# The first expert of an attention-and-experts kernel: six staging buffers for w1, token gathers right behind them, DVE makes the low halves

## The reference

```python
def _attn_ref(r, k, v, w, u):                 # B, H, S, D = 4, 8, 768, 48
    for t in range(S):
        kt, vt, rt = (k[:, :, t], v[:, :, t], r[:, :, t])
        cur = np.einsum('bhd,bhe->bhde', u[None] * kt, vt)
        y[:, :, t] = np.einsum('bhd,bhde->bhe', rt, state + cur)
        state = w[None, :, :, None] * state + np.einsum('bhd,bhe->bhde', kt, vt)

def _moe_ref(x, w_gate, w1, w2):              # N, D, E, F = 3072, 384, 8, 1024
    cap = N // E
    flat = (x @ w_gate).flatten()
    for idx in np.argsort(-flat):
        tok, e = (int(idx) // E, int(idx) % E)
        if assigned[tok] >= 0 or counts[e] >= cap:
            continue
        assigned[tok] = e
        counts[e] += 1
    for e in range(E):
        mask = assigned == e
        out[mask] = np.maximum(x[mask] @ w1[e], 0.0) @ w2[e]

def _moe2_ref(x, w_a, w_b, w_out):            # d_ff = 1536
    return (x @ w_a) * (x @ w_b) @ w_out
```

## Time and profile before

| | us |
|---|---|
| median of 3 executions | 904.5 |
| lowest and highest | 902.1, 906.38 |
| profiled execution, its own time | 903.44 |
| its span, first to last instruction | 901.5 |
| PE busy, share of the span | 831.6, 92% |
| DVE, ACT, POOL busy | 538.3, 234.6, 425.8 |

### The profile page before, as it was taken

One profiled execution on the slowest core, in us unless ns is written; L12 is line 12 of the kernel. 1 busy time (PEld: TensorE's weight loads), 2 busy tenths in 40 slices (PEclk: granted clock), 3 DMA queues, 4 the chain that ended last, 5 costly groups with the idle time before them and its releaser, 6 DMA issues.

```text
span 901.5 us, 19288 instructions
## 1 busy us (share of the span) xinstructions
PE 831.6 (92%) x7941; PEld 798.6 (89%) x7941; DVE 538.3 (60%) x1294; ACT 234.6 (26%) x494; POOL 425.8 (47%) x448
## 2 busy tenths in 40 slices
PE   5898987329999999999999999999999999999994
PEld 5798887219999999999999999999999999999994
DVE  6675765657776676677657675777576422631221
ACT  2233322021223123312322232223222222331221
POOL 5666764067047605751673177217622770475001
PEclk9999999559999999999999999999999999999998
DMA  9997951031012102210121122012101220121000
GB/s 171 204 226 169 223 134 47 1 113 55 1 59 80 55 1 71 77 46 14 66 79 37 36 65 67 27 36 80 54 27 36 88 59 12 60 82 53 1 1 27
DMA packets 94023, 61.82 MB, mean 69 GB/s; under 512 B 79344, under 2 KB 83952, under 8 KB 93936
## 3 DMA queue, kind: packets, MB, share of 16 engines
q0 software_dynamic: 11008, 34.61, 12.5%
q1 hardware_dynamic: 78640, 21.25, 11.9%
q10 hardware_dynamic: 4288, 4.72, 1.5%
HBM read 51.13 MB, written 9.44 MB: 67 GB/s over the span
## 4 chain that ended last, share of the span: by engine, by line
PE 76%; DVE 3%; issue 1%; DMA 1%; POOL 1%; ACT 0%; ACTq 0%; POOLq 0%; DVEq 0%
PE bank L1252 41%; PE bank L1326 17%; PE bank L1295 11%; PE bank L1308 2%; PE bank L1275 2%; PE bank L1312 1%; DVE mask_mem L682 1%; PE bank L1192 1%; DMA wst<-in_moe_w,rows_i 1%; PE bank L1243 1%; PE bank L1208 1%; PE bank L1200 1%; PE bank L1233 0%; POOL w L502 0%; DVE cand L678 0%
## 5 line engine op out<-in xcount | busy, mean ns | idle before, releaser
L1252 PE MATMUL bank<-act,w_all 128*128 128x384 f32 x1584 | 295.9, 338 | 0.0
L1252 PEld LDWEIGHTS bank<-act,w_all 128*128 128x128 f32 x1584 | 275.3, 188 | 0.0
L485 POOL DMA_INDIRECT wst<-in_moe_w,rows_i x48 | 52.3, 1090 | 246.3 <-DVE rows_i L752 190.9
L1326 PE MATMUL bank<-w_all,gs 128*128 128x384 f32 x864 | 167.4, 337 | 0.3 <-DVE gs L875 0.3
L502 POOL TENSOR_TENSOR w<-wst,w 128x384 fp32r<-128x384 f32 (+1 forms) x106 | 130.6, 1232 | 43.9 <-ACT w L1016 38.2
L1326 PEld LDWEIGHTS bank<-w_all,gs 128*128 128x128 f32 x864 | 150.0, 188 | 0.6 <-DVE gs L875 0.6
L1295 PE MATMUL bank<-hs,w 128*128 128x384 f32 x576 | 113.1, 340 | 0.0
L872 DVE TENSOR_TENSOR ga<-ga,bank 128x384 f32<-128x384 f32 x96 | 53.0, 552 | 86.2 <-PE bank L1252 80.6
L1295 PEld LDWEIGHTS bank<-hs,w 128*128 128x128 f32 x576 | 100.6, 188 | 0.0
L1037 ACT ACTIVATE gs<-ga 128x384 fp32r<-128x384 f32 x96 | 50.5, 526 | 187.2 <-DVE ga L872 187.2
L1252 PE MATMUL bank<-act,w 128*128 128x384 f32 x504 | 98.5, 339 | 0.0
(11 more groups left out here) (179 smaller groups left out, 1047.0 us busy)
## 6 DMA issues: line engine op xcount, KB each, us to landing
kt<-in_k SPq DMA_DIRECT2D x24, 192.0 KB, 4.1
rt<-in_r SPq DMA_DIRECT2D x24, 192.0 KB, 4.7
vt<-in_v SPq DMA_DIRECT2D x24, 192.0 KB, 4.9
x_rows<-xs ACTq DMA_DIRECT2D x24, 192.0 KB, 3.4
raw<-in_moe_w_a SPq DMA_DIRECT2D x6, 384.0 KB, 4.8
raw<-in_moe_w_b SPq DMA_DIRECT2D x6, 384.0 KB, 5.3
raw<-in_moe_w_out SPq DMA_DIRECT2D x6, 384.0 KB, 5.2
wst<-in_moe_w,rows_i POOLq DMA_INDIRECT x112
```

The source lines that it names most:

```text
L485: pool.indirect_dma_start(wst[:, k % STAGES, :], None, w1_rows, bass.IndirectOffsetOnAxis(ap=rows_i[:, k:k + 1], axis=0)).then_inc(wst_lan ...
L1252: last = pe.matmul(dst, wt(a), mv(b), start=(n == 0 and (a, b) == (0, 0)), stop=(n == len(pairs) - 1 and (a, b) == (1, 0)))
L1326: last = pe.matmul(acc[t][:, 0:D], gs2[:, c % 2, a, t * P:t * P + P], wo2[:, b, c, :], start=(c == 0 and (a, b) == (0, 0)), stop=(c == FFC ...
```

## The change

- `parts_of` gives blocks k = 3, 4, 5 of expert 0 staging buffers of their own: two stretches of `os_` and one of `ga`, with their own semaphores (`spare_landed`). Expert 0 thus has six buffers for its w1 blocks. The blocks of w2 go to `wst` as before; k = 6, 7, 8 wait for the low halves of 0, 1, 2.
- POOL's work for expert 0 is a function of its own, `prepare_first`: 16 increments of the semaphore `pool_go` (`PAD`), the wait for the row numbers, six gathers of w1, the three token gathers, then the gathers of w2, with POOL's halves of k = 8 on.
- DVE makes the low halves of k = 0 to 7 (before: 2 to 7): 0 to 5, then `route_keys(1)` and `lower_tokens(0)`, then 6 and 7. ACT's upper halves of the tokens come after k = 5 (before: after 4).
- The last three instructions of `route_places` become `route_close`, called ahead of `route_ids`, for every expert.
- DVE's two memsets after the attention stand ahead of the wait for the logits. In the last step of the attention ACT copies the logits of tile 22 ahead of the store of tile 23.

The diff, with what is only renamed left out:

```diff
+        spare_landed = [sem(f"spare_landed{n}") for n in range(STAGES)]
...
-        TOKENS_AT_0, TOKENS_AT = 4, 6
+        TOKENS_AT = 6
...
-        BY_DVE, BEFORE_TOKENS = range(2, 8), range(2, 5)
+        BY_DVE, BEFORE_TOKENS = range(0, 8), range(0, 6)
...
+        os_flat = os_[:, :, :].rearrange("p t d -> p (t d)")
+        spare = [os_flat[:, 0:WIDE], os_flat[:, WIDE:2 * WIDE],
+                 ga[:, :, :].rearrange("p q t -> p (q t)")[:, 0:WIDE]]
+        def in_spare(m, k):
+            return m == 0 and STAGES <= k < W1C
...
             def gather_weights(m, k):
-                if k >= STAGES:
+                if m == 0 and W1C <= k < W1C + STAGES:
+                    pool.wait_ge(w_split, 1 + (k - W1C + 1))
+                elif k >= STAGES and not in_spare(m, k):
                     pool.wait_ge(w_split, 1 + (m * CHUNKS + (k - STAGES + 1)))
                 else:
                     pool.wait_ge(w_split, 1 + m * CHUNKS)
...
+            def prepare_first():
+                for _ in range(PAD):
+                    pool.sem_inc(pool_go, 1)
+                pool.wait_ge(rows_ready, 1)
+                for k in range(W1C):
+                    gather_weights(0, k)
+                gather_tokens(0)
+                for k in range(W1C, CHUNKS + 2):
+                    if k < CHUNKS:
+                        gather_weights(0, k)
+                    if k - 2 > BY_DVE[-1]:
+                        split_weights(0, k - 2)
...
             dve.wait_ge(s_cpool, CP_ALL + 1)
-            dve.wait_ge(lg_ready, NT)
             dve.memset(is_open[:, :], 1.0)
             dve.memset(lid[:, :], BIG).then_inc(hole_step, 1)
             dve.wait_ge(hole_step, 1)
+            dve.wait_ge(lg_ready, NT)
...
+            def route_close(m):
                 dve.tensor_tensor(is_open[:, :], is_open[:, :], member[:, :], ALU.subtract)
                 link(m, dve.tensor_scalar(chosen[:, :], chosen[:, :], -2.0 * BIG, None, ALU.mult))
...
                     if more and c == 4 + PARTS:
+                        route_close(i + 1)
                         route_ids(i + 1)
...
             for part in range(PARTS):
                 route_slots(0, part)
+            route_close(0)
             route_ids(0)
             for k in BY_DVE:
                 if k == BEFORE_TOKENS[-1] + 1:
                     route_keys(1)
                     lower_tokens(0)
-                if k == BY_DVE[0]:
-                    dve.wait_ge(w_split, 1 + k)
...
                 upper_raw(n)
+                if n == NT - 1:
+                    copy_logits(n - 1)
                 store(n)
                 if n + 1 < NT:
                     copy_sums(n + 1)
-                if n >= 1:
+                if 1 <= n < NT - 1:
                     copy_logits(n - 1)
...
+PAD = 16
```

More of the change, by code:

```diff
@@ L325, in parts_of, with landings, landed @@
                 c, o = k * WIDE // F, k * WIDE % F
-                return wst[:, s, :], w1_2[:, 0, c, o:o + WIDE], w1_2[:, 1, c, o:o + WIDE]
+                return (spare[s] if in_spare(m, k) else wst[:, s, :],
+                        w1_2[:, 0, c, o:o + WIDE], w1_2[:, 1, c, o:o + WIDE])
             return wst[:, s, 0:D], w2_2[:, 0, k - W1C, :], w2_2[:, 1, k - W1C, :]
+        def landings(m, k):
+            s = k % STAGES
+            if m == 0:
+                return 16 * (k // STAGES if k >= W1C else 1)
+            return 16 * (m * len(range(s, CHUNKS, STAGES)) - 1 + k // STAGES + 1)
+        def landed(m, k):
+            return spare_landed[k % STAGES] if in_spare(m, k) else wst_landed[k % STAGES]
         CP_IDENT, CP_CAUSAL, CP_ALL = 4, 9, 29
@@ L502, in split_weights, with gather_tokens, prepare @@
                 pool.tensor_tensor(lo, src, hi.bitcast(F32), ALU.subtract).then_inc(w_split, 1)
-            def prepare(m, first):
+            def gather_tokens(m):
+                pool.wait_ge(ids_ready, m + 1)
+                pool.wait_ge(xg_turned, 1 + m * DC)
+                pool.sem_inc(pool_go, 1)
+                for t in range(CT):
+                    pool.indirect_dma_start(xg[:, t, :], None, x_rows,
+                                            bass.IndirectOffsetOnAxis(ap=ids_next[:, t:t + 1], axis=0)
+                                            ).then_inc(xg_landed[t], 16)
+            def prepare_first():
+                for _ in range(PAD):
+                    pool.sem_inc(pool_go, 1)
+                pool.wait_ge(rows_ready, 1)
[7 more added lines that the diff above has]
+                        split_weights(0, k - 2)
+            def prepare(m):
                 pool.wait_ge(rows_ready, m + 1)
@@ L510, in prepare @@
                         gather_weights(m, k)
[L511 to L518, removed]
-                                                    bass.IndirectOffsetOnAxis(ap=ids_next[:, t:t + 1], axis=0)
-                                                    ).then_inc(xg_landed[t], 16)
+                    if k >= 2:
+                        split_weights(m, k - 2)
+                    if k == TOKENS_AT:
+                        gather_tokens(m)
             def store(i):
@@ L530, in store @@
                 pool.sem_inc(o_flushed, 1)
[L532 removed]
+            prepare_first()
             for i in range(E - 1):
[L534 removed]
+                prepare(i + 1)
                 store(i)
@@ L1010, in upper_weights @@
             def upper_weights(m, k):
-                s = k % STAGES
-                uses = len(range(s, CHUNKS, STAGES))
-                act.wait_ge(wst_landed[s], m * (16 * uses) + 16 * (k // STAGES + 1))
-                src, hi, lo = parts_of(k)
+                act.wait_ge(landed(m, k), landings(m, k))
+                src, hi, lo = parts_of(m, k)
                 act.activation(hi, src, ACT.Copy).then_inc(w_hi, 1)
```

27 lines of the change are left out of this document (13 added, 14 removed).

## The result

| | before | after |
|---|---|---|
| median, us | 904.56 (4 executions) | 899.21 (4 executions) |
| lowest and highest | 902.1, 906.38 | 898.99, 900.08 |
| profiled execution, its span | 903.44, 901.5 | 899.0, 897.0 |

The ratio is 0.9944, 95% interval 0.992 to 0.9969: 5.35 us, 0.6%, faster. The forecast was 898.9 in a range of 896.8 to 901.6.

The account below looks back on a forecast made before the run. TensorE's back-to-back expert work bounds the kernel, so gains lie ahead of the first product: 0.65 + 0.13 + 0.54 + 4.28 = 5.60 us off the 904.5 median gives 898.9, range 896.8 to 901.6.

Parts of the forecast that it names:

- What bounds: TensorE busy 677.82 of 680 us in the experts; time saved ahead of the first product comes off the end nearly whole.
- Rival D: Expert 0: the start moves but the gain is lost to late w2 halves or search lists; 904 us, chance 0.05.
- Parts 1 and 2: End of attention: last logit copy ahead of the last store saves 0.65 us, memsets ahead of the logit wait 0.13.
- Part 3: First routing: `route_close` moved behind the third one-hot takes 0.54 us off the path to the token numbers.
- Part 4: POOL, before expert 0's first gather: 16 increments move a code load into idle time; row numbers to gather 1.08, not 3.69.
- Rival A: POOL's pad does nothing and the stall stays: tokens 1.22 us later, gain 4.4, 900.1 us; chance 0.20.
- Part 5: Expert 0's gathers: six buffers and new order bring the third token gather 5.60 us earlier, 4.28 from POOL's queue.
- Does DVE disturb the gathers?: POOL's six w1 gathers: even stretched by 0.19 or 0.23 us each beside DVE instructions, no cost.
- Third token gather to first product: Landing, transposes and halves of the tokens before expert 0's first product: taken as fixed at 4.93 us.
- B: Rival: w1 landings bunch, binding from 1.75 us spacing; at 1.89 costs 0.7 us, 899.6 us; chance 0.09.
- C: Rival: w1 blocks and tokens share DMA engines, landing over 2.9 us apart; slower, 907 us at 3.4; chance 0.04.
- The clock: First product: TensorE's clock rises 3.2 us after dense work; at once wins 1.6 us, twice as long loses 1.6.

Follow-up runs that it names:

- pad0: Changed kernel without the 16 semaphore increments on POOL (PAD = 0): median 899.20 us, ratio to before 0.9985.
- pad1: Changed kernel with one semaphore increment on POOL instead of 16: 896.55 us, one execution.
- pad129: Changed kernel with 129 semaphore increments on POOL instead of 16: 895.98 us, one execution.
- psum_numbers: Changed kernel with the first routing's one-hots reading the slot numbers from a PSUM bank instead of SBUF: median 896.52 us, ratio to before 0.9945.
- close_back: Changed kernel with route_close(0) back ahead of the one-hots of the first routing: 894.65 us, one execution.
- after: The changed kernel itself, against the kernel before: median 899.21 us, ratio 0.9944.
- after_again: The changed kernel, unedited, measured and profiled again: median 897.21 us, ratio to before 0.993.
- pad128: Changed kernel with 128 semaphore increments on POOL instead of 16: 900.42 us, one execution.
- warm: Changed kernel with token gathers ahead of gather k=5, plus some 120 extra identity matmuls on TensorE in the first routing: median 903.07 us, ratio to before 0.9995.

## Why the prediction was right, step by step

- **What bounds.** Held: 678.62 of 680 us busy, and the time ahead of the first product came off the end. Rival D (lost in expert 0) is out.
- **Parts 1 and 2**, 0.78: 0.80 measured, where the clock is high at the end of the attention. The profiled execution of the changed kernel has nothing of it.
- **Part 3**, 0.54: from row numbers to the end of `ids_next` it is 9.32 instead of 10.00, so 0.68, of which 0.31 is the last instruction itself (0.16 instead of 0.47), which I hadn't forecast. The one-hots do start 0.54 sooner. What counts is less, at most some 0.2, because the token gathers didn't wait for these numbers alone.
- **Part 4**, the pad: 1.23 from row numbers to first gather against 1.08 predicted, and the cause was right. **Its price was the worst term.** Rival A gave 1.22 for a pad without effect; it is 3.9. The step that failed is "POOL is free at 186.7, a microsecond before the token numbers": its sixth gather ended at 188.77, and these were ready at 187.34.
- **Part 5**, 4.82 with part 3: the measured 4.27 falls short by 0.55, and the token gathers are where. I had the first 0.85 behind `ids_next`; it was 1.73, since two gathers were held (0.83 and 1.02 above 0.95) and the sixth ended 1.43 us after the token numbers. From the first token gather to the third it was 2.51, not 2.69, and the numbers themselves came 0.14 sooner: 0.88 - 0.18 - 0.14 = 0.56. "Does DVE disturb the gathers?" was answered from gathers that stood beside short instructions; the one-hots of 1.2 us, to which the change moved the gathers, were not among them.
- **Third token gather to first product**, taken as fixed at 4.93: 4.92.
- **The landings** (B and C): they didn't bunch. The sixth block was in ACT's hands 3.56 us after its gather's start (187.57 to 191.13), the first 3.67, and from the first to the sixth it is 8.21 us at ACT and 8.32 at the issue, with unequal steps between. That is 1.64 a block, not the 1.28 I had counted on and not far from the 1.75 at which B binds, but it comes from the held gathers. So k=5 came at 191.13 and not 189.4, the keys ended at 194.70 and not 193.2, and the spare time before the tokens' lower half was 1.1 and not 2.2.
- **The clock**: it rose some 5.3 us after the first product's start, not 3.2. The 2.1 us more at half speed are worth about 1.05, within the 1.6 I gave; the end shows 0.74 more. The other traces say that the clock has less to do with it: where it rose 3.0 to 3.5 us after the first product's start (`pad0`, `pad1`, `pad129`, `psum_numbers`, `close_back`) it is 700.1 to 700.5 from there to the end, where it rose 5.3 to 5.5 after (`after`, `after_again`, `pad128`) 700.5 to 700.7. What makes the rest of the 0.74 stays open.
- **The number**: luck had a part. Both errors go the same way, 0.55 less gained before the first product and 0.74 lost behind it, and the profiled pair shows 4.50 and not 5.60. That the medians differ by 5.35 is the scatter of whole executions, so the time was met closer than the terms deserve.

## What to carry to other kernels

Two changes that both shorten one queue are priced together: in the trace the one alone took 2.11 us off the way to the first product, the other 0.39, both 4.27, since the second only pays once the first has emptied the queue ahead of it. (In whole times each alone was 0.15%, no more than noise, and both 0.6%.) When work is moved, look at which long two-input VectorE instructions it will then stand beside, not at what it stood beside before. A stall in "issue" just ahead of a gather may be a load of that engine's code. The signs here were a packet of the engine's instruction queue inside the stall, and a stall that went away with one cheap instruction in the idle time ahead of the wait and came back with 128. Where it falls moves with edits to that engine's program.

## What the runs showed of the hardware

- POOL's code came in pieces of 8 KB, 128 instructions. The first gather waited 2.4 us where a cut fell on the wait ahead of it (pads of 0 and 128); increments crossed a cut at their 0.08 us (pads of 16, 128 and 129).
- A gather that starts inside a one-hot of DVE with two SBUF inputs ends 0.8 us after it (1.78 to 1.97 us instead of 0.95 where it starts early in the one-hot); with one input in PSUM it takes 0.94 to 0.95.
- Gathers of 256 KB that nothing holds go out every 1.26 us. Most are in ACT's hands 3.3 to 3.9 us after their start, a few after 4.3 to 4.7 (the third of the kernel before, 185.38 to 190.11), held ones after 4.2 to 5.1. The sixth in a row took no longer than the first by more than 0.1 (3.56 and 3.67 in the changed kernel, 3.72 and 3.62 in `psum_numbers`).
- TensorE was granted the low clock through 32 us in which it was busy 29.33, in the one execution of `warm` that was profiled.
